# A block of attention, low-rank mixing and two feed-forward layers: attention done by pairs of heads, with host-turned queries and keys

## What is computed

```python
scores = scale * np.matmul(q, k.transpose(0, 1, 3, 2))
keep = is_global | is_local          # key < 8, or 0 <= query - key < 96
bias = -slopes[:, None, None] * dist[None, :, :]     # slope 2**-(h+1)
a = softmax(where(keep, scores + bias, -1e9));  x = a @ v
# heads side by side: x is 2 x 768 x 512
h = x.T @ U @ V                      # U 768x32, V 32x768, over positions
u = x + h.T
y = u + np.maximum(u @ w_ch1, 0.0) @ w_ch2           # 512 -> 2048 -> 512
xk, xr = mixtures of y and of y one position earlier, by mu_k and mu_r
out = sigmoid(xr @ w_r) * ((np.maximum(xk @ w_k, 0.0) ** 2) @ w_v)
```

## Time and profile before

| | us |
|---|---|
| median of 3 runs | 591.89 (590.57 to 592.38) |
| the profiled execution | 591.0 |
| its span in the profile | 589.3 |
| PE busy | 569.2 (97%) |
| DVE busy | 245.1 (42%) |
| POOL busy | 279.1 (47%) |
| ACT busy | 166.2 (28%) |

### The profile page before, as it was taken

One profiled execution on the slowest core, in us unless ns is written; L12 is line 12 of the kernel. 1 busy time (PEld: TensorE's weight loads), 2 busy tenths in 40 slices (PEclk: granted clock), 3 DMA queues, 4 the chain that ended last, 5 costly groups with the idle time before them and its releaser, 6 DMA issues.

```text
span 589.3 us, 10275 instructions
## 1 busy us (share of the span) xinstructions
PE 569.2 (97%) x3401; PEld 539.0 (91%) x3401; DVE 245.1 (42%) x681; ACT 166.2 (28%) x379; POOL 279.1 (47%) x289
## 2 busy tenths in 40 slices
PE   2999899999999999999999999999999999999997
PEld 1889899977999999999999999999999899898896
DVE  5788788875522222222222221222243153254123
ACT  2766667734411111111111111111232132221221
POOL 6645564208620008000596008793089599589100
PEclk9999999999999999999999999999999999999999
DMA  5587876234230003100055000000000100100101
GB/s 107 124 185 156 145 167 154 68 103 124 77 130 0 0 0 96 47 0 0 3 167 185 0 0 0 0 1 0 1 1 1 53 0 0 53 0 10 44 0 53
DMA packets 50084, 33.25 MB, mean 56 GB/s; under 512 B 39688, under 2 KB 39696, under 8 KB 50064
## 3 DMA queue, kind: packets, MB, share of 16 engines
q1 hardware_dynamic: 47504, 26.72, 16.9%
q10 hardware_dynamic: 2560, 6.29, 4.7%
HBM read 23.57 MB, written 3.15 MB: 45 GB/s over the span
## 4 chain that ended last, share of the span: by engine, by line
PE 81%; DVE 9%; DMA 4%; issue 3%; ACT 1%; DVEq 1%; POOL 0%; ACTq 0%; SPq 0%; POOLq 0%
PE bank L594 23%; PE bank L606 23%; PE bank L636 11%; PE bank L645 11%; PE bank L660 6%; DMA q_lh<-q_hl 3%; DVE probs L885 2%; PE bank L580 2%; DVE probs_t L896 2%; PE bank L477 2%; PE bank L499 2%; DVE x_nat L911 1%; PE bank L440 1%; PE bank L423 1%; DMA k_nat<-in_k 1%
## 5 line engine op out<-in xcount | busy, mean ns | idle before, releaser
L1064 DVE SCALAR_TENSOR_TENSOR HL<-bank,HH 128x384 fp32r<-128x384 f32 x64 | 35.7, 558 | 172.0 <-ACT HH L801 172.0
L801 ACT ACTIVATE HH<-bank 128x384 fp32r<-128x384 f32 x64 | 31.5, 492 | 231.2 <-PE bank L594 231.2
L1191 POOL TENSOR_SCALAR w1h<-raw 128x2048 fp32r<-128x2048 f32 x5 | 9.6, 1917 | 164.8 <-PE bank L606 140.8
L594 PE MATMUL bank<-UH,w1h 128*128 x256 | 86.3, 337 | 0.0
L606 PE MATMUL bank<-HL,w2h 128*128 128x384 f32 x256 | 86.1, 336 | 0.0
L594 PE MATMUL bank<-UH,w1l 128*128 x256 | 86.0, 336 | 0.0
L594 PE MATMUL bank<-UL,w1h 128*128 x256 | 85.9, 335 | 0.0
L606 PE MATMUL bank<-HH,w2h 128*128 128x384 f32 x256 | 85.8, 335 | 0.0
L606 PE MATMUL bank<-HH,w2l 128*128 128x384 f32 x256 | 85.8, 335 | 0.0
L718 ACT ACTIVATE probs<-probs,neg_max 128x256 f32<-128x256 f32 (+1 forms) x96 | 41.9, 486 | 31.7 <-DVE neg_max L885 29.9
L1082 DVE TENSOR_TENSOR k_square<-k_relu 128x384 f32<-128x384 f32 x32 | 23.4, 731 | 65.2 <-ACT k_relu L815 65.2
(11 more groups left out here) (128 smaller groups left out, 1241.0 us busy)
## 6 DMA issues: line engine op xcount, KB each, us to landing
raw<-in_moe_w_ch SPq DMA_DIRECT2D x8, 1024.0 KB, 5.2
q_lh<-q_hl ACTq DMA_DIRECT2D x32, 192.0 KB, 3.2
q_nat<-in_q SPq DMA_DIRECT2D x16, 192.0 KB, 4.1
k_nat<-in_k SPq DMA_DIRECT2D x16, 192.0 KB, 4.5
v_all<-in_v SPq DMA_DIRECT2D x16, 192.0 KB, 3.0
out<-result SPq DMA_DIRECT2D x12, 256.0 KB, 2.1
raw<-in_moe_w_v SPq DMA_DIRECT2D x2, 1024.0 KB, 5.3
raw<-in_moe_w_k SPq DMA_DIRECT2D x2, 1024.0 KB, 5.1
```

What stands on the lines that cost most here:

```text
L594: mm = pe.matmul(bank[4 + f % 2][:, 0:BLK], w[:, kt, f * P:(f + 1) * P], x[:, kt, ds(blk * BLK, BLK)], start=kt == 0 and n == 0, stop=kt = ...
L801: act.activation(HH[:, f % 2, :], bank[4 + f % 2][:, 0:BLK], ACT.Relu).then_inc(hid_high, 1)
L1064: dve.scalar_tensor_tensor(out=HL[:, f % 2, :], in0=bank[4 + f % 2][:, 0:BLK], scalar=0.0, in1=HH[:, f % 2, :].bitcast(F32), op0=ALU.max, ...
```

## The change

q and k reach the kernel turned, as 8 pairs of heads x 128 rows (64 channels of one head, 64 of the other) x 768 positions; v as one piece for each pair. The fills, ACT's window copies, the split of q and k, and the swap DMAs are gone. POOL now scales q (`prepare_qk`) and copies the window parts of k in `k_in`. A unit is two query tiles of both heads of a pair: 24 units of 4 column blocks for each head (3 in a pair's first). Its two heads use two whole banks, and the turned probabilities go to the banks that held the scores.

`scores` has a float32 product for each tile and head, with 64 rows; `weigh` has two float32 products for each block, each with 64 queries and 66 columns, into the two halves of bank 6's partitions. DVE copies the turned probabilities of one head, ACT those of the other. `sums_of_x`, `mixed` and their copies are done for each pair, in parts 0, 1 and 2, one part for each unit from unit 6 on (`piece`); the last pair's parts stand between the products of the first block of the first feed-forward layer. POOL splits the result into `UH` and `UL`. The loads of the first two weight chunks stand near the start, their splits in POOL's first two pairs. Attention is written out unit by unit, without loops. The first layer's products and all of the second layer stay.

On SP:

```diff
-            for h in range(3):
-                load_qk(h)
...
+            def load_qk(p):
+                sp.dma_start(q_in[:, p % 2, :], qt[p]).then_inc(qk_in[p % 2], 16)
+                sp.dma_start(k_in[:, p % 2, 4:10, :].rearrange("p t n -> p (t n)"), kt_[p]).then_inc(qk_in[p % 2], 16)
+            def load_v(p):
+                sp.dma_start(v_in[:, p % 2, :, :, 0:D], vp[p]).then_inc(v_landed[p % 2], 16)
...
+            for p in range(2, PAIRS):
+                sp.wait_ge(qk_done, UNITS * (p - 1))
+                sp.wait_ge(qk_in[p % 2], 32 * (p // 2))
+                load_qk(p)
+                sp.wait_ge(pv_done, UNITS * (p - 1))
+                sp.wait_ge(v_landed[p % 2], 16 * (p // 2))
+                load_v(p)
```

On PE:

```diff
+            def scores(n):
+                p, u = n // UNITS, n % UNITS
                 if u == 0:
+                    pe.wait_ge(q_scaled, p + 1)
+                    pe.wait_ge(k_past, 2 * p + 2)
+                if n >= 3:
+                    for i in range(2):
+                        pe.wait_ge(ptevac[i], n - 2)
+                for t, at, w in unit_tiles(u):
+                    for h in range(2):
+                        r = slice(h * D, (h + 1) * D)
+                        mm = pe.matmul(bank[UNIT_BANKS[n % 3][h]][:, at:at + w].rearrange("p (a n) -> p a n", n=P),
+                                       q_in[r, p % 2, t * P:(t + 1) * P], window(p % 2, r, t), start=True, stop=True)
...
+            def weigh(n):
+                p, u = n // UNITS, n % UNITS
+                if n >= 1:
+                    pe.wait_ge(norm_done, n)
...
+                            for r in (slice(0, P // 2), slice(P // 2, P)):
+                                mm = pe.matmul(bank[O_BANK][r, (2 * i + h) * DV:(2 * i + h + 1) * DV],
+                                               probs_t[:, n % 2, h, c * P + r.start:c * P + r.stop], src,
+                                               start=c == places[0], stop=c == places[-1])
...
+            def mixed(p, half):
+                if half == 0:
+                    pe.wait_ge(a_ready, 2 * (p + 1))
+                    pe.wait_ge(v4_step, 2)
+                else:
+                    pe.wait_ge(y_kept, 2 * p + 1)
+                to = bank[M_BANK]
+                pe.matmul(to[:, 0:BLK], A4[:, p % 2, :], V4[:, half * BLK:(half + 1) * BLK], start=True, stop=False)
+                for i in range(TPB):
+                    mm = pe.matmul(to[:, i * P:(i + 1) * P], pair_x(p, half * TPB + i), ident[:, :],
+                                   is_transpose=True, start=False, stop=i == TPB - 1)
...
+                for n in range(NU + 3):
+                    if n < NU:
+                        scores(n)
+                    if 2 <= n < NU + 2:
+                        turn(n - 2)
+                    if piece(n):
+                        mixing(*piece(n))
+                    if n >= 3:
+                        weigh(n - 3)
```

On ACT:

```diff
+            def mixing(p, part):
+                if part == 0:
+                    act.wait_ge(a_done, p + 1)
+                    act.activation(A4[:, p % 2, :], bank[M_BANK][:, 0:P], ACT.Copy).then_inc(a_high, 1)
                     return
...
+                act.wait_ge(mix_done, 2 * p + part)
+                act.activation(Y[:, kt, 2 * (p // PPB) + part - 1, 1:BLK + 1], bank[M_BANK][:, 0:BLK],
+                               ACT.Copy).then_inc(y_kept, 1)
...
+                for n in range(NU + 3):
+                    if n < NU:
+                        exps(n)
+                    if 2 <= n < NU + 2:
+                        evac(n - 2)
+                    if piece(n):
+                        mixing(*piece(n))
```

On DVE:

```diff
+                for n in range(NU + 3):
+                    if n < NU:
+                        maxima(n)
+                    if piece(n) and piece(n)[1] == 1:
+                        a_low(piece(n)[0])
+                    if 2 <= n < NU + 2:
+                        evac(n - 2)
+                    if n >= 3:
+                        normalise(n - 3)
```

On POOL, where `prepare_qk(0)` stands ahead:

```diff
+                prepare_qk(1)
+                prepare_v(0)
+                prepare_v(1)
+                factors()
+                for p in range(PAIRS):
+                    if p + 2 < PAIRS:
+                        prepare_qk(p + 2)
+                    if p >= 1:
+                        split_u(p - 1, 0)
+                        split_u(p - 1, 1)
+                    if p + 2 < PAIRS:
+                        prepare_v(p + 2)
+                    if p < 2:
+                        split_chunk(p)
```

More of the change, by code:

```diff
@@ L219, in block_kernel @@
         pt_done = sem("pt_done")
-        ptevac_done = sem("ptevac_done")
+        ptevac = [sem(f"ptevac{i}") for i in range(2)]
         pv_done = sem("pv_done")
@@ L497, in sums_of_x @@
+                mm.then_inc(pv_done, 1)
+            def sums_of_x(p):
+                pe.wait_ge(norm_done, UNITS * (p + 1))
+                if p == 0:
                     pe.wait_ge(u4_set, 1)
-                for t in range(first, last):
-                    mm = pe.matmul(bank[b][:, :], U4[:, t, :, :].rearrange("p a r -> p (a r)"),
-                                   x_nat[:, t, b * H:(b + 1) * H, :].rearrange("p h d -> p (h d)"),
+                else:
+                    pe.wait_ge(y_kept, 2 * p)
+                for t in range(ST):
+                    mm = pe.matmul(bank[M_BANK][:, 0:P], U4[:, t, :, :].rearrange("p a r -> p (a r)"), pair_x(p, t),
@@ L589, in hidden @@
+                for p in range(PAIRS - 1):
+                    for part in range(3):
+                        mixing(p, part)
             def hidden(Q, blk, f, w1h, w1l):
@@ L721, in v4_high @@
-            def v4_high():
-                act.wait_ge(uv_in, 80)
-                act.activation(V4[:, :], v4_raw[:, :], ACT.Copy).then_inc(v4_step, 1)
-            def pair(p):
-                for n in range(6):
-                    s, u = n // 3, n % 3
-                    if is_last(p) and n == 3:
-                        v4_high()
-                    exps(p, n)
-                    for part in ahead(p, n):
-                        evac(*part)
-                    if u == 2 and ahead(p, n):
-                        swap(2 * p + s + 2, s)
@@ new lines, in _, with relu @@
+                for p in range(PAIRS - 1):
+                    for part in range(3):
+                        mixing(p, part)
+            def relu(step, f):
+                act.wait_ge(hid_done, FQ * step + f + 1)
+                if f == 1:
+                    act.wait_ge(acc_done, KT * step + KT)
+                else:
+                    act.wait_ge(hid_used, (FQ - 1) * step + max(f - 1, 0) + 1)
+                act.activation(HH[:, f % 2, :], bank[4 + f % 2][:, 0:BLK], ACT.Relu).then_inc(hid_high, 1)
@@ L1060, in _ @@
+            low_half(0, 0)
+            low_half(0, 1)
+            a_low(PAIRS - 1)
+            low_half(0, 2)
+            low_half(0, 3)
+            dve.wait_ge(u_ready, 2 * PPB)
+            add_to_y(0, 0)
+            dve.wait_ge(u_ready, 2 * PAIRS)
+            with dve.Fori(1, NBLK) as blk:
+                for f in range(FQ):
+                    low_half(blk, f)
+                add_to_y(blk, blk)
+            with dve.Fori(1, NQ) as Q:
                 with dve.Fori(0, NBLK) as blk:
```

1080 lines of the change are left out of this document (442 added, 638 removed).

## The result

The changed kernel takes 565.64 us (median of 4 runs, 562.01 to 566.67), the kernel before 592.0 beside it on the same chip: a ratio of 0.9548, with a 95% interval of 0.9503 to 0.9593. The profiled execution took 566.67 us, its span is 564.9. The forecast was 578 (560 to 606). So it is faster, as forecast, by 26.4 us where 14 were forecast.

The account below looks back on a forecast made before the run. PE bounds the kernel, with DVE also near full in attention. Start 17.1, three units 13.0, six pairs 95.4 and tail 10.5 put the first layer at 136.0, 16.6 earlier; less 2.6 mixing, net -14.0: 578 us (560 to 606).

Parts of the forecast that it names:

- The start: Before the pairs: keys land turned, first scores at 8.0 us, scores(3) at 17.1, unit 6 at 30.1.
- Scores: Eight float32 records a unit on half rows: the two heads run side by side, 1.07 us.
- The rival with 1.72: Score products: half rows don't run side by side, 1.72 us a unit, execution 595 us; chance 0.20.
- Value records: Products in `weigh`: 32 records of 66 columns with half the weight columns, 0.06 us each, 1.9 us a unit.
- 0.11 as the rival: Products in `weigh`: each record keeps the 0.11 us of a full weight load, execution 612 us; chance 0.14.
- the ring: Next scores wait for ACT's copy behind four exponentials: 4.6 us for a full unit, 3.9 for a pair's first.
- Changes of shape: Array going between full rows, half rows and half columns, three times a unit: 0.16 us each, lower bound nothing.
- The wait for `a_low`: Part 1: PE stands at the mixed product until DVE's `a_low`, behind four maxima, at 3.5 us; part 6.0 us.
- POOL: slack: POOL has 5 us of work in a 15.9 us pair; one to three units of slack around its weight splits.
- The last units: End of attention: three units without scores, PE alone, 10.5 us, first layer begins at 136.0.
- The jumps of the loops: Attention written out without loops: their jumps go, and they cost nothing before, as PE streams through them.
- The clock rival: PE idles some 1.5 us in each part 1; the lower clock returns, about +70 us, 650; chance 0.05.

Follow-up runs that it names:

- the run with both orders: Changed kernel with TensorE's mixing moved behind its value products and ScalarE's copy moved between the two heads' exponentials: 554.21 us, ratio 0.9395.

## Why the prediction was right, and where its sizes were off

**The start: right in the sum, in part by luck.** First scores at 8.97 (forecast 8.0), scores(3) at 17.00 (17.1), unit 6 at 30.02 (30.1). Keys are ready 1 us later than I estimated, and the three units behind them take that much less; two errors cancel.

**Scores: right, size and reason.** 1.09 us with the change of shape, forecast 1.07 and 0.16. The records of the two heads start almost together, as the prediction named for a sign, and each holds its rows for 0.21 us. Only "about 5 of the 8 record times" was too many: it is four, 0.86 us, and the change of shape. The rival with 1.72 is refuted.

**Value records: the term that was mis-sized.** The step was "I take 0.06", with 0.11 as the rival and 0.055 as the lower bound of a record that streams alone. It is 0.029: each record takes its 0.055, and two run at a time. The prediction allowed for that overlap between heads in the scores and did not take it for the two halves of the columns here. In part 0 that is 24 x 0.031 = 0.7 us less, in part 1 32 x 0.031 = 1.0; in part 2 the ring covers it. So 1.7 of the 2.6 us between 15.9 and 13.3 are this one term. The rest is the faster maxima (four in part 1, 0.2; two in the ring of part 2, 0.1), ScalarE's copy in part 2 (384 columns in 0.38 us, priced as 512 in 0.60), and the changes of shape that stand inside a wait and cost nothing there; the mixed block takes 0.27 more than forecast. The prediction had named the possibility ("below 0.055, if the two halves overlap"), but took 0.06, half of a full record. The pairs alone gained 15.6 us over the forecast; the end of the branch took 7.4 back.

**Changes of shape: right.** Eight turns at 0.107 are 0.86, the chain has 1.02; 32 value records at 0.029 are 0.93, the chain has 1.08. So a change costs 0.15 to 0.16 us, the value that I took. On this the Trainium skill (TensorEngine Tiling (Array Packing), Key Properties) and the trace agree that a change has a price, and it is small beside what the half-size records save.

**The wait for `a_low` and the ring through ACT: right.** I priced part 1 at 6.0 and part 2 at 4.5, without changes of shape; they take 5.13 and 4.14, less by the cheaper value records and four maxima (0.345 instead of 0.40) in part 1, and by two maxima and the shorter copy in part 2. The runs that move the mixing and the copy take away just these waits, 0.9 us in part 1 and 0.7 in part 2.

**POOL: slack right for this kernel.** It is gone once a pair takes some 12 us, as the run with both orders shows.

**The last units** took 9.0 us instead of 10.5. The value records save 88 x 0.031 = 2.7 us there; longer sums (1.58 us, not 1.3), longer mixed blocks and 0.8 us in which TensorE stands for `a_low` and for `x_nat` take part of it back.

**What I missed.** "The jumps of the loops go, and cost nothing now." I looked at the jumps that went and not at the one that stayed: the end of the attention branch. In the kernel before, TensorE goes from its sums to the next ones without a pause there (18 records in 7.75 us), and the record of its branch is short:

```profile
L528 PEldq COMPARE_BRANCH  x2: 89/201/313, 7.3 to 128.7; - x2
```

0.31 us, against 3.5 to 5.1 in the changed kernel and the later runs that leave the first branch. So the old jump was not hidden behind queued work, it was itself short, and nothing in the profile before showed a price. The changed kernel pays 4.5 us for the jump and 2.9 us for the clock behind it. Its fallback is longer (266 matrix products are written there for TensorE, 102 before); that this is the reason was not tried.

**The clock rival (5 in 100): not in the pairs,** where the granted clock is 1.00 over all 79.8 us, though TensorE stands for 1.2 us in each part 1. It did come after the longer stop at the end, for 18 records.

**The sum from the measured terms:** 575.3 forecast for the span, less 15.6 for six pairs and 1.5 for the last units, plus 4.5 for the jump and 2.9 for the clock, less 0.7 (mixing inside the first block costs 438.6 - 436.7 = 1.9, not 2.6) is 564.9, the span of the profile.

## What to carry to other kernels

Where TensorE is the bound and a change uses parts of its array, price the record by its own rows and columns (0.21 and 0.055 us here), count two halves at a time, and keep one at a time as a rival. To test whether things run side by side, changing the order in the kernel is not enough; read the starts in the trace, because the order may not be kept. When a stretch of code is written out unit by unit, look at what the engine jumps over when it leaves it, and at the record of its branch: an alternative branch that never runs cost 7 us here. And in a ring of four engines, move the instruction that nobody waits for behind the one that somebody does: two such moves gave 11.4 us here, over 4 tenths of what the change itself gave.

## What the runs showed of the hardware

- Float32 records on the two halves of the rows run side by side: a record of 256 columns holds its 64 rows for 0.21 us, and two start within 0.01 to 0.02 us of each other. The order in the kernel doesn't matter (1.09 and 1.10 us for eight): TensorE starts a product of the second half ahead of one of the first that stands before it.
- The same holds for the two halves of the stationary columns: two records with 64 stationary and 66 moving columns cost 0.058 us together, one with 128 stationary columns 0.108.
- A change between such shapes costs 0.15 to 0.16 us in the stream.
- The custom maximum over 256 columns takes 0.34 us with the slope as a number and 0.41 with the slope in memory.
- TensorE's branch over the fallback lasts 3.5 to 5.1 us when it leaves the first of two branches and 6.0 to 6.2 when it enters the second; in the kernel before it lasts 0.31. Of 3.6 us, 36 records queued ahead hid two thirds, and a second stop of 2.7 us came behind it.
- After a stop of 4.5 us the granted clock reads 0.50 over the next 3 us; after stops of 1.2 us in every pair it stays at 1.00.
